# Attention's output laid over two PSUM banks at row 64, with one set of v products, and the 1e-9 of the softmax sums added by ACT

## The reference, cut to what matters

```python
B, H, S, D = 2, 8, 576, 64
scores = scale * q @ k.T;  scores[causal] = -1e9
a = exp(scores - scores.max(-1))
a /= a.sum(-1) + 1e-09
local = a @ v
q_p = phi(q)                                  # where(q > 0, q, exp(q) - 1) + 1
mem_out = (q_p @ M_prev) / (q_p @ z_prev + 1e-6)
attn = g * mem_out + (1 - g) * local          # g = sigmoid(beta), per head
x = attn as [1152, 512]
g = where(h >= 1, h, where(h <= -1, 0, (h + 1)**2 / 4)) of h = x @ w_in   # [512, 2048]
x2 = g @ w_out                                # [2048, 512]
# then top-1 routing over 8 experts with capacity 288 and two products per expert
```

## Time and profile before

| what | value |
|---|---|
| median of 3 runs | 307.69 us (306.95, 307.69, 309.27) |
| profiled execution | 307.44 us, of it 305.3 us span |
| PE busy | 297.8 us (98%), 2821 instructions |
| DVE busy | 217.4 us (71%), 583 instructions |
| ACT busy | 151.4 us (50%), 332 instructions |
| POOL busy | 136.4 us (45%), 154 instructions |
| granted TensorE clock | full in all 40 slices of the span |

### The profile page before, as it was taken

One profiled execution on the slowest core, in us unless ns is written; L12 is line 12 of the kernel. 1 busy time (PEld: TensorE's weight loads), 2 busy tenths in 40 slices (PEclk: granted clock), 3 DMA queues, 4 the chain that ended last, 5 costly groups with the idle time before them and its releaser, 6 DMA issues.

```text
span 305.3 us, 7256 instructions
## 1 busy us (share of the span) xinstructions
PE 297.8 (98%) x2821; PEld 247.5 (81%) x2821; DVE 217.4 (71%) x583; ACT 151.4 (50%) x332; POOL 136.4 (45%) x154
## 2 busy tenths in 40 slices
PE   7999999999999999999999999999999999999993
PEld 6666676676666988887999998999989898996863
DVE  3999998999978367897885557955785559880520
ACT  1796866867766244655551444345344546501110
POOL 4878997998998300373782003003312334020031
PEclk9999999999999999999999999999999999999999
DMA  8999798861537700000000407751015019349980
GB/s 164 158 207 228 191 203 174 192 172 46 166 68 206 228 5 0 2 2 0 2 0 2 77 2 287 266 90 30 0 20 93 7 18 384 150 124 392 354 320 9
DMA packets 75047, 38.48 MB, mean 126 GB/s; under 512 B 66008, under 2 KB 66016, under 8 KB 73988
## 3 DMA queue, kind: packets, MB, share of 16 engines
q1 hardware_dynamic: 72340, 36.74, 45.8%
q10 hardware_dynamic: 2416, 0.59, 1.0%
q0 software_dynamic: 256, 0.67, 0.6%
HBM read 32.66 MB, written 5.39 MB: 125 GB/s over the span
## 4 chain that ended last, share of the span: by engine, by line
PE 94%; POOL 2%; DVE 1%; issue 1%; ACT 0%; POOLq 0%
PE bank_a L1841 17%; PE bank_b L1841 17%; PE bank_out L1798 6%; PE bank_a L1697 4%; PE bank_b L1901 4%; PE bank_pt L1901 4%; PE bank_pt L1749 4%; PE bank_a L1775 3%; PE bank_out L1795 2%; PE bank_a L2080 2%; PE bank_out L1874 2%; PE bank_b L2080 2%; PE bank_b L1692 2%; PE bank_out L2189 2%; PE bank_out L1786 2%; PE bank_a L2090 2%
## 5 line engine op out<-in xcount | busy, mean ns | idle before, releaser
L720 POOL TENSOR_SCALAR prob<-prob,rl,gate_loc 128x512 f32<-128x512 f32 (+3 forms) x64 | 41.5, 662 | 11.0 <-DVE rl L1230 11.0
L1841 PE MATMUL bank_a<-x_hi,win_hi 128*128 128x288 f32 x128 | 39.3, 307 | 0.0
L1841 PE MATMUL bank_b<-x_hi,win_hi 128*128 128x288 f32 x128 | 38.2, 298 | 0.0
L1841 PE MATMUL bank_b<-x_lo,win_hi 128*128 128x288 f32 x128 | 38.0, 297 | 0.0
L1841 PE MATMUL bank_b<-x_hi,win_lo 128*128 128x288 f32 x128 | 38.0, 297 | 0.0
L1841 PE MATMUL bank_a<-x_hi,win_lo 128*128 128x288 f32 x128 | 38.0, 297 | 0.0
L1841 PE MATMUL bank_a<-x_lo,win_hi 128*128 128x288 f32 x128 | 37.9, 296 | 0.0
L972 ACT ACTIVATE g_raw<-bank_a,biases 128x576 f32<-128x576 f32 x16 | 11.9, 742 | 49.5 <-DVE sq L1310 49.5
L909 ACT ACTIVATE prob<-prob,negmax 128x512 f32<-128x512 f32 (+3 forms) x64 | 35.0, 549 | 0.3 <-DVE negmax L1180 0.3
L804 POOL TENSOR_TENSOR w_lo<-w_sb,w_hi 128x512 fp32r<-128x512 f32 x8 | 11.4, 1426 | 48.2 <-ACT w_hi L1015 48.2
L749 POOL TENSOR_TENSOR x_lo<-xT,x_hi 128x1152 fp32r<-128x1152 f32 x4 | 10.6, 2662 | 48.6 <-ACT x_hi L922 48.6
(11 more groups left out here) (322 smaller groups left out, 792.2 us busy)
## 6 DMA issues: line engine op xcount, KB each, us to landing
w_sb<-in_moe_w_dram SPq DMA_DIRECT2D x6, 2048.0 KB, 12.0
win_raw<-in_moe_w_in_dram SPq DMA_DIRECT2D x4, 1024.0 KB, 5.6
wout<-in_moe_w_out_dram SPq DMA_DIRECT2D x4, 1024.0 KB, 6.1
win_raw<-in_moe_w_in_dram SPq DMA_DIRECT2D x1, 4096.0 KB, 13.6
out_dram<-zero_row SPq DMA_DIRECT2D x8, 288.0 KB
x_d<-x_rows SPq DMA_DIRECT2D x32, 72.0 KB, 2.1
v_sb<-in_v_dram SPq DMA_DIRECT2D x16, 128.0 KB, 2.5
qn<-in_q_dram SPq DMA_DIRECT2D x24, 72.0 KB, 5.4
```

The costliest lines, as they stand in the source:

```text
L720: pool.tensor_scalar(prob[u][:, h, :], prob[u][:, h, :], rl[:, c:c + 1], gate_loc[:, 2 * j + h:2 * j + h + 1], ALU.mult, ALU.mult).then_in ...
L1841: last = pe.matmul(h_bank(d)[:, t, :], w[:, m, f:f + P], x[c % 2][:, m, :], start=(m == 0 and n == 0), stop=(m == KT - 1 and n == 2))
```

## The change

Four things are changed together.

1. The output lies from column `X_AT` = 448 of `bank_out` on, so that rows 0 to 63 are the last 64 columns of `bank_t` and rows 64 to 575 fill `bank_o`. The rows from 128 c on of tiles c = 1, 2, 3, and 512 to 575 of tile 4, then lie in one bank: one product each. Only tile 0 needs two, 0 to 63 and 64 to 575. The tiles of the memory part move with it: the first has 64 rows, the other four 128 (`mem_tile`).
2. On PE the end of a pass is add_memory(j), memory(r), values(j), with all products in values, behind the wait for copy 6.
3. The addition of 1e-9 is an ACT instruction (`row_sums`) on the row sums, with a bias of 1e-9 from the third column of `biases`. It stands behind `below_zero(r + 1)` for part 0 and behind the last exponential for part 1 (of pair 0, at the start of r = 1). DVE keeps the reciprocal and waits for it.
4. In r = 2 to 6, `turn_k(r + 1)` stands behind `row_max(r, 4)` on DVE, in place of the start of the pass.

```diff
+        X_AT = NFULL * P - TAIL
+        def mem_tile(t):
+            at = max(0, TAIL + (t - 1) * P)
+            return at, P if t else TAIL
...
-                pool.wait_ge(s_rl, 4 * j + (2 if u in (2, 3) else 4))
+                pool.wait_ge(s_rl, 2 * j + (1 if u in (2, 3) else 2))
...
+            def row_sums(i, part):
+                cols = slice(0, 4) if part == 0 else slice(4, 9)
+                act.wait_ge(s_exp, 5 * i + (2 if part == 0 else 5))
+                act.activation(rl[:, cols], rsum[:, cols], ACT.Identity, bias=biases[:, 2:3]).then_inc(s_eps, 1)
...
-                act.activation(xT[:, j, :], bank_out[:, 0:S], ACT.Copy).then_inc(s_xe, 1)
+                act.activation(xT[:, j, :], bank_out[:, X_AT:X_AT + S], ACT.Copy).then_inc(s_xe, 1)
...
                 if r == 1:
                     exp_s(0, 4)
+                    row_sums(0, 1)
...
                     exp_s(r, 2)
                     if 0 < r < NPAIR - 1:
                         below_zero(r + 1)
+                    row_sums(r, 0)
                     exp_s(r, 1)
...
                     if r > 0:
                         exp_s(r, 4)
+                        row_sums(r, 1)
...
             def row_factor(i, part):
                 cols = slice(0, 4) if part == 0 else slice(4, 9)
-                dve.wait_ge(s_exp, 5 * i + (2 if part == 0 else 5))
-                dve.tensor_scalar(rl[:, cols], rsum[:, cols], 1e-9, None, ALU.add).then_inc(s_rl, 1)
-                dve.wait_ge(s_rl, 4 * i + 2 * part + 1)
+                dve.wait_ge(s_eps, 2 * i + part + 1)
                 dve.reciprocal(rl[:, cols], rl[:, cols]).then_inc(s_rl, 1)
...
                 if 1 < r < NPAIR - 1:
                     turn_q(r + 1)
-                    turn_k(r + 1)
...
                     row_max(r, 4)
+                if 1 < r < NPAIR - 1:
+                    turn_k(r + 1)
                 if r < NPAIR - 1:
                     phi(r + 1)
...
             def add_memory(j):
...
-                    pe.matmul(bank_out[:, t * P:t * P + w], mem[j % 2][0:w, t, :, :].rearrange("p h d -> p (h d)"), ident[0:w, 0:w],
-                              is_transpose=True, start=(t in (0, NFULL)), stop=False)
+                    at, w = mem_tile(t)
+                    pe.matmul(bank_out[:, X_AT + at:X_AT + at + w], mem[j % 2][0:w, t, :, :].rearrange("p h d -> p (h d)"),
+                              ident[0:w, 0:w], is_transpose=True, start=(t < 2), stop=False)
...
             def values(j):
                 pe.wait_ge(s_v[j % 2], 48 * (j // 2 + 1))
-                add_memory(j)
                 copied(j, 2)
                 copied(j, 5)
-                for c in reversed(range(NFULL)):
-                    times_v(j, c, False)
-
-            def last_values(j):
                 copied(j, 6)
-                for c in range(NT):
-                    last = times_v(j, c, True)
+                for c, q0, q1 in ((3, 3 * P, S), (2, 2 * P, S), (1, P, S), (NFULL, NFULL * P, S), (0, 0, TAIL), (0, TAIL, S)):
+                    w = P if c < NFULL else TAIL
+                    for h in range(2):
+                        last = pe.matmul(bank_out[D * h:D * h + D, X_AT + q0:X_AT + q1], v_sb[j % 2][0:w, c, h, :],
+                                         probT[0:w, h, c * KSTEP + q0:c * KSTEP + q1], start=False, stop=(c == 0))
                 last.then_inc(s_pv, 1)
...
-                if r > 0:
-                    values(j)
-                if 0 < r < NPAIR:
-                    memory(r)
...
                 if r > 0:
-                    last_values(j)
+                    add_memory(j)
+                if 0 < r < NPAIR:
+                    memory(r)
+                if r > 0:
+                    values(j)
```

More of the change, by code:

```diff
@@ L101, in build_program @@
         iota_hi, _, _ = sb("iota_hi", [ST, E], F32)
-        biases, _, _ = sb("biases", [P, 2], F32)
+        biases, _, _ = sb("biases", [P, 3], F32)
         tok_f, _, _ = sb("tok_f", [ST, N // ST], F32)
@@ L307, in build_program @@
         s_exp = sem("s_exp")
+        s_eps = sem("s_eps")
         s_rl = sem("s_rl")
@@ L693, in _ @@
             pool.memset(biases[:, 0:1], 0.5)
+            pool.memset(biases[:, 2:3], 1e-9)
             pool.memset(biases[:, 1:2], -1.0).then_inc(s_const, 1)
@@ L937, in _ @@
                     copy_x(r - 2)
+                if r == 0:
+                    act.wait_ge(s_const, 1)
                 if r == 1:
                     exp_s(0, 4)
+                    row_sums(0, 1)
                 if r > 0:
@@ L1772, in memory @@
                 for t in range(NT):
+                    at, w = mem_tile(t)
                     for h in range(2):
                         part = slice(D * h, D * h + D)
-                        last = pe.matmul(mem_bank(i)[0:rows[t], t, h, :], qpT[i % 2][part, t * P:t * P + rows[t]], mz[part, i, :],
-                                         start=True, stop=True)
+                        last = pe.matmul(mem_bank(i)[0:w, t, h, :], qpT[i % 2][part, at:at + w], mz[part, i, :], start=True, stop=True)
                 last.then_inc(s_nm, 1)
@@ L1784, in add_memory @@
                 for t in range(NT):
-                    w = rows[t]
-                    pe.matmul(bank_out[:, t * P:t * P + w], mem[j % 2][0:w, t, :, :].rearrange("p h d -> p (h d)"), ident[0:w, 0:w],
-                              is_transpose=True, start=(t in (0, NFULL)), stop=False)
[L1789 to L1800, removed]
+                    at, w = mem_tile(t)
+                    pe.matmul(bank_out[:, X_AT + at:X_AT + at + w], mem[j % 2][0:w, t, :, :].rearrange("p h d -> p (h d)"),
+                              ident[0:w, 0:w], is_transpose=True, start=(t < 2), stop=False)
             def values(j):
                 pe.wait_ge(s_v[j % 2], 48 * (j // 2 + 1))
-                add_memory(j)
                 copied(j, 2)
                 copied(j, 5)
-                for c in reversed(range(NFULL)):
-                    times_v(j, c, False)
-            def last_values(j):
                 copied(j, 6)
-                for c in range(NT):
-                    last = times_v(j, c, True)
+                for c, q0, q1 in ((3, 3 * P, S), (2, 2 * P, S), (1, P, S), (NFULL, NFULL * P, S), (0, 0, TAIL), (0, TAIL, S)):
[3 more added lines that the diff above has]
+                                         probT[0:w, h, c * KSTEP + q0:c * KSTEP + q1], start=False, stop=(c == 0))
                 last.then_inc(s_pv, 1)
@@ L1964, in keep_running @@
                 for i in range(n):
-                    at = (NT + i % 2) * P
+                    at = S + i % 2 * P
                     pe.transpose(bank_out[:, at:at + P], ident[:, :], ident[:, :])
```

## The result

The changed kernel takes 311.90 (median of 4 runs, 310.98 to 313.15) against 307.75 of the kernel before beside it: a ratio of 1.0139, 95% interval 1.0112 to 1.0167. Measured again on another occasion it took 310.93 against 307.61, ratio 1.0095 (1.0063 to 1.0127). So the change costs 3.3 to 4.2, where +0.2 was forecast. The profiled execution took 310.98 with a span of 309.2, 3.9 longer than before's.

The account below looks back on a forecast made before the run. PE was taken to bound the attention stage, busy 11.99 of 11.99 in a pair. From 307.44, -1.44 + 1.36 + 0.15 + 0.1 = +0.2 gave 307.6; forecast range 306.4 to 308.6 (chance 0.60), 8 in 10 for 305.2 to 310.0.

Parts of the forecast that it names:

- The transposes of the memory part keep their five instructions, only the short one comes first; nothing: Memory-part transposes on PE: same five instructions with the short one moved first, priced at no change.
- The signs of being wrong: PE waiting every pair for last copy or row maximum; pairs shrinking over 0.35; r = 1 gap under 0.5 or over 2.5.
- Products at 3.00 against 3.18: Products of v on PE: 24 instructions a pair, 12 fewer, save 0.18 a pair, 1.44 for 8.
- The wait in r = 1, +1.36: PE before memory(1): waits 1.56 for phi(1), held by ACT's addition, against 0.20 before; 1.36 lost once.
- The clock in the new gap, chance 0.02: Rival, PE's gap in r = 1: the granted clock falls, each pair at half clock costing up to 12; chance 0.02.
- The reciprocal stalls behind POOL, 0.12: Rival, DVE in five pairs: POOL's subtraction holds the reciprocal, products wait; up to 2.8, so 310.4; chance 0.12.
- phi(1) meets POOL, 0.08: Rival, r = 1: POOL's scaling goes first, memory(1) comes 0.33 to 0.8 later, 307.9 to 308.4; chance 0.08.
- The row maximum in front of memory, +0.15: PE before memory(r), 6 pairs: waits 0 to 0.05 a pair for the last row maximum; 0.15 taken.
- The last copy in r = 6, +0.1: Products in r = 6: ACT also splits x there, priced at 0.1 of waiting.
- turn_k moved and SP's queue, nothing: DVE and SP: later turn_k has slack enough, loads of v pushed by some 2 are not needed yet; no cost.
- It does not do what it says: Rival, products of v: they save nothing, giving 308.9; chance 0.03.
- The signs named ahead: Trace after: 24 product instructions for about 3.0, pair 11.8, one PE wait near 22, reciprocals 0.18, copies before products, ACT additions 0.18.

Follow-up runs that it names:

- experiment 2: Changed kernel with the 64-row tile last in add_memory, memory and the products: 309.33 against 307.97 for the kernel before, ratio 1.0030.
- 4: Changed kernel with the short tile last in every group and, in r = 1, phi(1) ahead of the row factor: 307.82 against 307.97, ratio 1.0016.
- experiment 6: Changed kernel with phi(1) early in r = 1, short tile last in add_memory and memory but first in the products: 306.65 against 307.61, ratio 0.9973.
- experiment 7: Kernel before with one edit, the products of the last rows taking the 64-row tile of v first: 306.94 against 307.76, ratio 0.9970.
- experiment 1: Kernel before with only ACT's 1e-9 addition and the later turn_k, PE's order and products unchanged: 307.62 against 307.97, ratio 0.9991.

## Why the prediction was wrong, step by step

- **The step that failed: "The transposes of the memory part keep their five instructions, only the short one comes first; nothing", and with it the order of the six pieces.** The costs of instructions were taken by count and columns, order left out. The short tile first costs the transposes 0.15 a pair (0.64 to 0.79), and fourth of six it costs the products 0.15 (3.00 to 3.15). That is 0.30 a pair, 2.4 over eight, and turns the forecast's -1.44 into a loss. Experiments 2 and 4 show it by taking it back; 6 and 7 show that the order has a price elsewhere too. The trace of before had the hint: its groups all had the short tile last, so none of its rows showed the price of another order. An unseen order should have been bounded from both sides, as the products' price was; it was costed at a flat nothing.
- **The signs of being wrong.** None of the three came: no wait in every pair, no pair shrunk by over 0.35, a gap in r = 1 of 1.46. Pairs that grow were not among them, so the list could not catch this miss.
- **Products at 3.00 against 3.18.** The sum of wide and narrow instructions was right where the short tile is last: 3.00 in experiment 2. The changed kernel's 3.15 is the point above.
- **The wait in r = 1, +1.36.** Right: 1.46 seen, 1.26 net of the old wait. ACT's instruction was under-priced (0.18 from the earlier trace rows, measured 282 to 301 ns), phi's path otherwise as written.
- **The clock in the new gap, chance 0.02.** The fall came far more often than that, in about half of the runs (4 of 8 by mean clock). Its price was over-stated: the granted clock is low for some 3.5 (0.87, 0.50 and 0.77 in three stretches of 2.00 in experiment 2's profile), not for a pair, and costs 1.6 each time. The earlier trace rows was read as evidence against, and the run of that stretch did not carry over. At 1.6 in about half of the runs it is some 0.8 of the mean.
- **The reciprocal stalls behind POOL, 0.12.** False: 164 to 190 ns for all 16 in the changed kernel, 0.16 inside a subtraction in experiment 1. This rests on the runs. The Trainium skill, "SBUF — State Buffer", section "Who interferes with whom", takes contention between DVE and GpSimd to come from their shared ports alone and names tensor_scalar, not the reciprocal, among those that can take them. The traces agree: at the same place the addition, a tensor_scalar, was held for 1.24, the reciprocal not.
- **phi(1) meets POOL, 0.08.** Did not come: POOL was not first. phi took 0.73, with POOL's scaling starting 0.19 behind it.
- **The row maximum in front of memory, +0.15.** Not there: PE has no such wait after. **The last copy in r = 6, +0.1.** There, about 0.2: 0.13 of waiting and 3.22 for 3.15.
- **turn_k moved and SP's queue, nothing.** Right, by experiment 1.
- **Two small slips in the working.** The last copy is 0.66 long in the earlier trace rows, not 0.6. The 308.9 of "It does not do what it says" is 307.44 + 1.44; by the prediction's own terms without the gain it is 307.44 + 1.36 + 0.15 + 0.1 = 309.05. Neither moves the forecast.
- **The signs named ahead.** 24 instructions for 3.0 (3.15), the pair at 11.8 (12.11), a wait of 1.5 near 22 (1.46 before 24.73). The pair's stretch missed by 0.3, and that times eight, 2.4, is the larger part of the miss of 3.1 to 4.0; the clock is most of the rest.

What stays open: what in the array makes a short tile dear. The idle 0.17 of the weight loads is seen on entering 64 rows from 128, but in the changed kernel's last pair a 128*64 load behind a 128*128 one (112.12) stands 0.17 idle as well. Nor does the number of changes between 64 and 128 rows give one price: two fewer of them are worth 0.12 (experiment 7), 0.15 (6) and 0.23 (2) a pair, and nothing in the last pair of experiment 6. That the gain of 6 and 7 comes from two halves of the array at work side by side fits all their rows, but no run was made to test it alone. And why the clock fell in one of ten runs of experiment 2 but in half of the changed kernel's, with nearly the same gap (1.6 and 1.46), was not settled.

## What to carry to other kernels

Where TensorE is the bound, the order of weight tiles of different heights is part of the price, and it has to be measured. Here the short one was cheapest at the end of its group, or first behind a short tile in the other half of the partitions; first behind a tall one it cost 0.15 more. Such a move, one line in the kernel before, is worth 0.3%. A step moved forward has to be checked in the first pass of a loop, where its producers stand elsewhere. And a TensorE gap in the middle of full work can cost more than its length: here a gap of 1.5 or more cost 1.6 on top in some runs, by the clock.

## What the hardware showed that was not expected

- Transposes of one 64-row and four 128-row tiles take 0.79 with the short one first and 0.64 with it last; products 3.15 with it fourth of six, 3.00 last. Where it is first behind memory's 64*64 tile, memory and products together take 4.22 against 4.37; first behind the transposes' 64-row tile, the products take 3.00.
- A product starts ahead of the two memory instructions that precede it in PE's list, 47.38 against 47.47 in experiment 6 and 49.56 against 49.65 in experiment 7. The product and those two lie in different halves of the partitions.
- The granted clock fell to 1.2 GHz behind single gaps of 1.5 to 1.6 in some runs, of 2.3 in all four, and was back within 4; in the profiles the products behind the gap took 1.6 to 1.7 longer.
- ACT takes 282 to 301 ns for 128x4 or 128x5 elements with a bias from SBUF, longer than DVE's 156 to 161 for the same addition unhindered.
- The first five transposes of the program take 0.64 in some profiled runs, 0.73 in one and 1.09 to 1.15 in others, of kernels with and without the change, at a granted clock shown as full.
